# Routed experts and a PReLU FFN on one core: the third routing's values read back by SyncE, a second bank for the FFN's second step, and the search passes at other steps

## What is computed

```python
def _moe_ref(x, w_gate, w1, w2):
    cap = N // E
    order = np.argsort(-(x @ w_gate).flatten())
    for idx in order:
        tok, e = (int(idx) // E, int(idx) % E)
        if assigned[tok] >= 0 or counts[e] >= cap:
            continue
        assigned[tok] = e
        counts[e] += 1
    for e in range(E):
        mask = assigned == e
        out[mask] = np.maximum(x[mask] @ w1[e], 0.0) @ w2[e]

def _moe2_ref(x, w_in, w_out, alpha):
    h = x @ w_in
    g = np.maximum(h, 0.0) + alpha * np.minimum(h, 0.0)
    return (g @ w_out).astype(np.float32)
```

## Time and profile before

| | |
|---|---|
| median of 3 runs | 1042.72 us (1041.45 to 1043.27) |
| the profiled execution | 1040.79 us, span 1039.1 us |
| TensorE busy | 96% |
| VectorE, ScalarE, GpSimd busy | 55%, 37%, 18% |
| mean granted TensorE clock | 0.992 of full |

### The profile page before, as it was taken

The page is one execution under the profiler, slowest core; times in us unless marked ns, Lnnn a source line. Parts: engine busy times, 40 slices in busy tenths (PEclk is TensorE's granted clock), DMA queues, the critical chain, the costliest instruction groups (busy, mean ns, idle before and its releaser), DMA issues.

```text
span 1039.1 us, 16704 instructions
## 1 busy us (share of the span) xinstructions
PE 998.8 (96%) x6533; PEld 857.1 (82%) x6533; DVE 572.7 (55%) x1299; ACT 389.3 (37%) x625; POOL 188.0 (18%) x202
## 2 busy tenths in 40 slices
PE   8999999988979999999999999999999999999997
PEld 5555555557978898799989998998999999989996
DVE  4444444598655827947953685496439537221112
ACT  5676676401341124356322224542222356122212
POOL 0010100105520011243301015350100335100001
PEclk9999999999989999999999999999999999999999
DMA  9999996407488685866877855679696436976601
GB/s 210 271 274 273 256 287 198 175 21 249 152 278 277 209 224 181 282 142 214 290 282 234 252 172 122 202 217 377 212 237 213 158 113 193 337 263 215 215 27 54
DMA packets 121476, 222.34 MB, mean 214 GB/s; under 512 B 51424, under 2 KB 69216, under 8 KB 121408
## 3 DMA queue, kind: packets, MB, share of 16 engines
q1 hardware_dynamic: 87152, 120.11, 37.3%
q0 software_dynamic: 21280, 91.59, 28.4%
q10 hardware_dynamic: 12976, 9.70, 3.9%
HBM read 184.84 MB, written 36.52 MB: 213 GB/s over the span
## 4 chain that ended last, share of the span: by engine, by line
PE 85%; DVE 9%; issue 2%; ACT 2%; DMA 1%; POOLq 0%; POOL 0%; DVEq 0%; ACTq 0%
PE psum L955 20%; PE psum L967 19%; PE psum L932 11%; PE psum L902 11%; PE psum L694 8%; PE psum L678 7%; DVE hits L1541 4%; PE psum L897 2%; PE psum L662 2%; PE psum L705 1%; PE psum L927 1%; DMA stage<-x_rows,tok_idx 1%; DVE unit L1441 1%; PE psum L849 1%; PE psum L713 1%
## 5 line engine op out<-in xcount | busy, mean ns | idle before, releaser
L955 PE MATMUL psum<-y_high,unit 128*128 128x448 f32 x768 | 230.9, 368 | 4.4 <-ACT below L1152 4.3
L967 PE MATMUL psum<-g_high,unit 128*128 128x448 f32 x756 | 227.8, 369 | 4.3 <-DVE g_low L1469 4.2
L955 PEld LDWEIGHTS psum<-y_high,unit 128*128 128x128 f32 x768 | 144.2, 188 | 17.9 <-ACT below L1152 5.8
L967 PEld LDWEIGHTS psum<-g_high,unit 128*128 128x128 f32 x756 | 142.0, 188 | 18.9 <-DVE g_low L1469 7.8
L955 PE MATMUL psum<-y_low,unit 128*128 128x448 f32 x384 | 140.3, 365 | 0.0
L1441 DVE TENSOR_TENSOR unit<-raw,unit 128x768 fp32r<-128x768 f32 (+1 forms) x106 | 109.9, 1059 | 51.5 <-ACT unit L1125 44.8
L967 PE MATMUL psum<-g_low,unit 128*128 128x448 f32 x378 | 138.2, 366 | 0.0
L1151 ACT ACTIVATE above<-psum 128x448 f32<-128x448 f32 x64 | 34.9, 545 | 248.8 <-PE psum L955 248.8
L932 PE MATMUL psum<-h_high,unit 128*128 128x224 f32 x672 | 118.5, 280 | 8.8 <-issue 8.8
L1464 DVE SCALAR_TENSOR_TENSOR below<-below,neg_alpha,above 128x448 f32<-128x448 f32 x64 | 43.8, 684 | 147.0 <-ACT below L1152 146.8
L902 PE MATMUL psum<-x_high,unit 128*128 128x224 f32 x672 | 117.3, 276 | 0.0
(11 more groups left out here) (184 smaller groups left out, 1319.4 us busy)
## 6 DMA issues: line engine op xcount, KB each, us to landing
unit<-ffn_parts SPq DMA_DIRECT2D x120, 768.0 KB, 6.7
ffn_parts<-pre_parts POOLq DMA_DIRECT2D x24, 768.0 KB, 6.7
ffn_parts<-unit SPq DMA_DIRECT2D x8, 768.0 KB, 5.5
q_in<-in_q_dram SPq DMA_DIRECT2D x24, 224.0 KB, 5.5
v_in<-in_v_dram SPq DMA_DIRECT2D x24, 224.0 KB, 7.5
x_rows<-x_tok POOLq DMA_DIRECT2D x8, 672.0 KB, 5.9
rank_in<-suit_flat POOLq DMA_DIRECT2D x6, 896.0 KB
k_in<-in_k_dram SPq DMA_DIRECT2D x23, 224.0 KB, 7.0
```

The lines of the kernel that those rows point to most:

```text
L955: last = pe.matmul(psum[:, IN_BANK, 0:PAIR], w, y[:, c, :], start=(c == 0 and i == 0), stop=(c == DC - 1 and i == 2))
L967: last = pe.matmul(psum[:, OUT_BANK + d, 0:PAIR], w, g[:, m % 2, :], start=(m == 0 and i == 0), stop=(m == (FC - 1 if q < GROUPS - 1 else ...
```

## The change

1. **Read-back by SP.** For routing 2 the store of `suit` and its read-back leave GpSimd's list. SP, between the attention's loads and the FFN's loads, waits for the values, stores them, waits for the store, waits until unit w2_unit(1, EC - 3), the sixth piece of routing 1's w2, has landed, and issues the read-back; `third_loaded` releases VectorE's first pass. GpSimd gathers all eight pieces of w2 one after the other. For routings 4 and 6 two gathers of w2 now stand between GpSimd's store and its read-back.
2. **Bank of the second w_in piece.** Piece 1 goes into bank OUT_BANK + DC - 1 = 6 and does not wait for `in_taken`. The first `ffn_out` of a group waits, before its last block of columns, until ScalarE has read that bank.
3. **Passes.** Other steps for the passes of routings 2, 3, 4 and 6, and for THR_AT, FLAGS_AT and IDX_AT of 2 and 3.

```diff
+        def in_bank(m):
+            return OUT_BANK + DC - 1 if m == 1 else IN_BANK
...
                 if r == 2:
-                    passes, later = (21, 22, 23, 29, 30, 31, 32, 33), (34, 35, 37, 41)
+                    passes, later = (21, 22, 23, 24, 25, 28, 30, 31), (33, 34, 36, 41)
                 elif r == 3:
-                    passes, later = range(45, 53), (54, 55, 57, STEPS + 5)
+                    passes, later = (42, 43, 44, 46, 48, 50, 51, 52), (54, 56, 58, STEPS + 5)
                 elif r % 2 == 0:
-                    passes, later = (9, 11, 13, 16, 22, 24, 28, 29), (31, 32, 34, 38)
+                    passes, later = (9, 11, 13, 16, 22, 24, 26, 28), (31, 32, 34, 38)
...
+            sp.wait_ge(suit_done, 3)
+            sp.dma_start(suit_flat[0].rearrange("e (p g) -> p e g", g=G), suit[:]).then_inc(third_stored, 16)
+            sp.wait_ge(third_stored, 16)
+            sp.wait_ge(*loaded(w2_unit(1, EC - 3)))
+            sp.dma_start(rank_in[:], suit_flat[0].unsqueeze(1).to_broadcast([E, DIGIT, P * G])).then_inc(third_loaded, 16)
...
-            store_suit(2)
-            gather_w2(1, range(3))
-            spread_suit(2)
-            gather_w2(1, range(3, EC))
+            gather_w2(1)
...
-                        repeat_suit(2 * q + 4)
-                    gather_w2(2 * q + 2, range(early, EC))
+                        store_suit(2 * q + 4)
+                    gather_w2(2 * q + 2, range(early, min(early + 2, EC)))
+                    if q < GROUPS - 2:
+                        spread_suit(2 * q + 4)
+                    gather_w2(2 * q + 2, range(early + 2, EC))
...
-                if m > 0:
+                if m > 1:
                     pe.wait_ge(in_taken, FC * q + m)
...
-                        last = pe.matmul(psum[:, IN_BANK, 0:PAIR], w, y[:, c, :],
+                        last = pe.matmul(psum[:, in_bank(m), 0:PAIR], w, y[:, c, :],
...
+                    if m == 0 and d == DC - 1:
+                        pe.wait_ge(in_taken, FC * q + 2)
...
-                        dve.wait_ge(rank_loaded, 16 * (r - 1))
+                        if r == 2:
+                            dve.wait_ge(third_loaded, 16)
+                        else:
+                            dve.wait_ge(rank_loaded, 16 * (r - 2))
```

More of the change, by code:

```diff
@@ L285, in attention_routed_moe_prelu_ffn @@
         rank_loaded = sem("rank_loaded")
+        third_stored = sem("third_stored")
+        third_loaded = sem("third_loaded")
         pre_loaded = [sem(f"pre_loaded{i}") for i in range(PRE_RING)]
@@ L609, in spread_suit @@
             def spread_suit(r):
-                wait(suit_stored, 16 * (r - 1))
+                wait(suit_stored, 16 * (r - 2))
                 pool.dma_start(rank_in[:], suit_flat[r % 2].unsqueeze(1).to_broadcast([E, DIGIT, P * G])
@@ L1150, in take_in @@
                 act.wait_ge(unit_used, in_unit(q, m) + 1)
-                act.activation(above[:, m % 2, :], psum[:, IN_BANK, 0:PAIR], ACT.Relu)
-                act.activation(below[:, m % 2, :], psum[:, IN_BANK, 0:PAIR], ACT.Relu, scale=-1.0).then_inc(in_taken, 1)
+                act.activation(above[:, m % 2, :], psum[:, in_bank(m), 0:PAIR], ACT.Relu)
+                act.activation(below[:, m % 2, :], psum[:, in_bank(m), 0:PAIR], ACT.Relu, scale=-1.0).then_inc(in_taken, 1)
             def round_g(q, m):
```

## The result

The changed kernel takes 1030.35 us (median, 1028.86 to 1030.82) against 1042.09 before: ratio 0.9889, interval 0.9866 to 0.9912. The profiled execution took 1028.86 us, span 1027.2. Faster, as forecast, with an interval clear of 1, but by 11.6 us instead of 19.6, and 0.85 us above the top of the range (1029.5).

The account below looks back on a forecast made before the run. TensorE, busy 96% of the span, was taken as the bound, with a 7.38 us hole and a lower clock behind it. Gains 6.5 + 3 x 1.85 + 1.3 + 6.2 = 19.6 us from 1042.72 gave 1023, range 1018.5 to 1029.5.

Parts of the forecast that it names:

- The hole and its cause: Before routing 1's second product: TensorE waits 7.38 us because the read-back delays w2 gathers; moving it starts the product 300.1.
- The store: SP's store of the values beside the x-row gather: delays those rows by 0 to 1.8 us, taken as 0.5.
- VectorE's work as the next thing late: Before the first FFN product: five passes, 15.55 us, put the y split at 319.0; 3.3 of 10.3 us given back.
- Bank and passes: FFN groups: second w_in piece in its own bank gains 1.85 us in groups 0, 1 and 2, 1.3 in group 3.
- rival A: Routing 2's read-back lands late, 302.3 to 307, costing 1 to 3 us; 1024 to 1026 alone, chance 0.17.
- 295 + 2 + 5.3: Read-back's landing at 302.3: sixth w2 piece at 295, 2 us of starting, 5.3 us of all engines.
- VectorE (303.4): Before the first search pass: VectorE is ready at 303.4, after its last h and w2 splits.
- The second support: Read-back length from the later read-back's 8 us beside other work in 378 to 386; would land at 307.
- rival E: SP's queue: read-back and FFN loads wait for the sixth piece, making it slower, 1043 to 1050 us; chance 0.03.
- the table's first line: Span up to the first FFN product: forecast gain 6.5 us, measured 2.0 (326.69 to 324.66).
- rival B: Clock falls at the new 3.3 us stall before the FFN, costing 1.5 to 3 us; chance 0.13.
- Part 3: Group 0's FFN: moved passes bring it to group 1's length but for 0.5, gaining 6.2 us.

Follow-up runs that it names:

- eight_reads: Changed kernel with SP's read-back cut into eight transfers of 16 partitions, one per expert; 1026.87 us, ratio 0.9865.
- two_all: Changed kernel with values stored twice and every read-back, GpSimd's too, as 16 rows each repeated 8 times; 1024.26 us, ratio 0.9848.
- bank_alone: Kernel before with the second bank alone, all passes where they were; 1039.74 us, ratio 0.9985.
- bank_passes: Kernel before with the second bank, and passes of routings 4 and 6 at 26 and 28 instead of 28 and 29; 1036.97 us, ratio 0.9959.
- move_alone: Kernel before with routing 2's read-back on SP, but one bank and the old pass tables; 1035.35 us, ratio 0.9933.
- probe_forms: Changed kernel plus four lone transfers before the read-back: 8 by 16 different rows 10.8 us, 16 by 8 6.7, one row 128 times 4.5, 128 different rows 4.5.
- probe_eight: Changed kernel plus three lone transfer sets: eight transfers of different rows 8.3 us, eight of repeated rows 9.2, the old single form 10.5.
- hold_loads: Changed kernel with SP's FFN loads held back until the read-back has landed; 1029.38 us, ratio 0.9883.
- three_first: Changed kernel with three instead of five passes of routing 2 ahead of the y split, the others and sums later; 1025.71 us, ratio 0.9843.
- two_copies: Changed kernel with values stored twice and read back as 16 rows each repeated 8 times, for routing 2 alone; 1024.53 us, ratio 0.9854.

## Why the prediction was right and wrong

**Right.** The hole and its cause: with the read-back out of GpSimd's queue the sixth piece landed by 293.3, the product went on at 300 and ended at 316.4, at full clock. The store cost next to nothing, as VectorE was ready at 303.5. VectorE's work as the next thing late: 15.6 us from the first pass to the split, and in `eight_reads` and `two_all`, where the values were there in time, a stop of 3.3 us to the tenth. Bank and passes: 1.85 and 1.3 a group reckoned; 1.95, 1.74 and 1.29 measured; and they need each other, as `bank_alone` and `bank_passes` show.

**Wrong: one duration.** The step that failed is rival A's "295 + 2 + 5.3", the length of the read-back, and with it the forecast's premise that VectorE (303.4) is later than the values. I took the length from its queue's share of the DMA engines (62.5% of 12 us less two gathers). A share over 16 engines says nothing on the length of a transfer that uses only half of the engines' time (0.50 to 0.52 in the probes): alone it takes 10 us, and 15 beside other transfers. Nor does the subtraction hold: the queue's 2.18 MB less 0.92 are three gathers of 0.39 MB, not two. The second support, 8 us in 378 to 386, left out the start. The read-back of routing 4 before the change was issued at 373.63, so by the same end it took 12.4 us:

```profile
373.63 0.64 POOL L611 DMA_DIRECT2D rank_in<-suit_flat  x1 [5.25 <-DMA suit_flat<-suit]
```

A length much nearer to the truth stood in the text: rival E has "at most 13.5 us", from 288.24 to 301.77. I used it to dismiss a slow case, and not to price the likely one. It is no bound, though, since 301.77 is the cast of the next gather and no use of the values, and 15.0 was measured. That 295 + 13.5 gives 308.5, where 308.35 was measured, is luck: the issue was 1.7 us earlier and the transfer 1.5 longer. As VectorE was ready at 303.5 after the last w2 split, 4.8 us were lost here, against A's 1 to 3; less what the store didn't cost, this is the 4.5 us missing in the table's first line.

**The clock, rival B**, came with it: 8.81 against 7.53 for the first 36 FFN matmuls, 1.3 us. It also fell with a stop of 3.3 us (`eight_reads`, `two_all`), so my forecast without it was wrong even by its own stop.

**Part 3** was too short in the same place. The values of routing 4 were reckoned 21.6 us after tok_idx, read from where the rate rose again. They took from 357.8 to 383.4, 25.6 us: the transfer 15.0 against 12.4, the store and the gathers before it some 1.4 more. (tok_idx itself was reckoned at 351.3 and came 6.5 us later, with the later FFN and its clock.) The pass at step 42 waited 2.4 us, and TensorE 0.9 and 0.7. 4.5, 1.3 and 1.6, with small change, make the 7.7 us that are missing. `two_all` has the first and the third back: its span is 16.8 us under the one before, where 19.6 were forecast. Of the 2.8 left, 1.6 are the clock and 0.8 are group 2; by the ratio it gains 15.8 us.

What the text did not weigh: two more passes ahead of the y split are worth 5.7 us as soon as the values are late, and 3.3 even when they are not. `move_alone` starts the FFN 3.9 us sooner than the full change.

## What to carry to other kernels

Bound the length of a transfer by the time from its issue to the first use of what it brings, never from its share of the engines or from work of another transfer; and look at the first dimension of a repeating read: 8 in front took 10 us, 16 took 6.7, a flat 128 took 4.5. When a wait goes, count how much of another engine's work now stands between the new last arrival and the next product, and move that work behind it. A second buffer brings its gain only if the work that lay in the old wait's shadow moves too.

## What the runs showed of the hardware

- The same 0.92 MB into the same 128 partitions took 4.5 to 10.8 us by the form of the transfer alone; reading one row 128 times cost nothing (`probe_forms`).
- Eight transfers into 16 partitions each kept all engines busy at 140 and 159 GB/s (`probe_eight`), where a flat one into 128 partitions moved 369 to 437 (`probe_forms`).
- The read-back took 15.0 us beside other traffic both from SP's queue and from GpSimd's. A gather of 0.39 MB issued with it or up to 0.5 us after it was cast 11.8 to 14.7 us after its issue (`hold_loads`, `three_first`, `move_alone`).
- The clock fell from the 2.4 to the 1.2 GHz level behind stops of 8.2 us (changed kernel), 5.3 (`hold_loads`), 3.3 (`eight_reads`, `two_copies`, `two_all`) and 2.2 (`move_alone`), and not behind one of 2.5 (`three_first`); each cost 1.3 to 1.7 us in the first FFN matmuls.
